# Attention rebuilt for a mixture-of-experts kernel: r and k loaded column-first, scores of a head pair on two 64-row halves of the array, x stationary in the gate

## The reference

```python
for t in range(S):
    cur = einsum('bhd,bhe->bhde', u * k[t], v[t])
    y[t] = einsum('bhd,bhde->bhe', r[t], state + cur)
    state = w * state + einsum('bhd,bhe->bhde', k[t], v[t])
```

## Time and profile before

| | us |
|---|---|
| median of 3 runs | 2269.34 (2267.15 to 2274.19) |
| the profiled execution, its span | 2269.7 |
| attention, to the first transfer of routing | 211.7 |
| TensorE busy in the first 212 us | 189.2 |
| VectorE, GpSimd, ScalarE busy there | 136.4, 105.3, 32.8 |

### The profile page before, as it was taken

How to read it: one execution, slowest core, us unless ns; L and a number is a source line. 1 busy time by engine, 2 the same in 40 slices (tenths; PEclk the granted TensorE clock), 3 DMA queues, 4 the chain that set the end, 5 groups by cost and what they waited for, 6 DMA issues and landing times.

```text
span 2269.7 us, 31806 instructions
## 1 busy us (share of the span) xinstructions
PE 2104.9 (93%) x12371; PEld 1901.0 (84%) x12371; DVE 819.8 (36%) x1525; ACT 470.7 (21%) x662; POOL 406.3 (18%) x258
## 2 busy tenths in 40 slices
PE   6996333999989999999999999999999999999998
PEld 6995322999978998998898899899899899889888
DVE  6676776222253223223223223222322322322322
ACT  0112000344412122113112211211221221212211
POOL 4555112555510011002000100200020020003011
PEclk9998555999999999999999999999999999999999
DMA  6453100233310001001000100100010000000000
GB/s 138 79 83 100 51 0 10 79 131 131 122 56 0 0 12 44 0 0 56 0 0 0 55 0 0 55 0 0 0 55 0 0 31 25 0 0 14 17 24 28
DMA packets 105473, 79.33 MB, mean 35 GB/s; under 512 B 77408, under 2 KB 96992, under 8 KB 105440
## 3 DMA queue, kind: packets, MB, share of 16 engines
q1 hardware_dynamic: 102368, 69.44, 11.1%
q0 software_dynamic: 3072, 9.44, 1.2%
HBM read 69.43 MB, written 9.44 MB: 35 GB/s over the span
## 4 chain that ended last, share of the span: by engine, by line
PE 71%; DVE 1%; issue 0%; POOL 0%; DVEq 0%
PE bank L1000 71%; DVE weight L1332 0%; PE bank L972 0%; PE bank L1215 0%; DVE row_sum L1318 0%; DVE x_lo L993 0%; PE bank L984 0%; DVE weight L1321 0%; DVE col_part L1323 0%; POOL out_dram L1307 0%; DVE row_sum L1320 0%; DVE col_inv L1328 0%; DVE col_inv L1331 0%; DVE x_rows L1362 0%; DVE row_sum L1319 0%
## 5 line engine op out<-in xcount | busy, mean ns | idle before, releaser
L1000 PE MATMUL bank<-x_hi,w_hi 128*128 128x512 f32 (+1 forms) x1344 | 524.2, 390 | 1.9 <-ACT x_hi L1079 1.2
L1000 PE MATMUL bank<-x_hi,w_lo 128*128 128x512 f32 (+1 forms) x1344 | 523.8, 390 | 0.0
L1000 PE MATMUL bank<-x_lo,w_hi 128*128 128x512 f32 (+1 forms) x1344 | 520.4, 387 | 0.0
L1000 PE MATMUL bank<-w_hi,h_hi 128*128 128x384 f32 x1536 | 519.4, 338 | 0.0
L1000 PE MATMUL bank<-w_hi,h_lo 128*128 128x384 f32 x1536 | 518.8, 338 | 0.0
L1000 PE MATMUL bank<-w_lo,h_hi 128*128 128x384 f32 x1536 | 518.8, 338 | 0.0
L1279 ACT ACTIVATE h_hi<-bank 128x512 fp32r<-128x512 f32 x384 | 229.7, 598 | 1190.3 <-PE bank L1000 1190.3
L1338 DVE SCALAR_TENSOR_TENSOR h_lo<-bank,h_hi 128x512 fp32r<-128x512 f32 x384 | 265.6, 692 | 557.6 <-ACT h_hi L1279 557.6
L144 POOL TENSOR_TENSOR w_lo<-w_raw,w_hi 128x3072 fp32r<-128x3072 f32 x16 | 109.3, 6831 | 1310.6 <-ACT w_hi L136 1310.6
L1362 DVE SCALAR_TENSOR_TENSOR x_rows<-bank,weight,x_rows 128x384 f32 (+1 forms) x192 | 118.4, 618 | 530.2 <-PE bank L1000 530.2
L1000 PEld LDWEIGHTS bank<-x_hi,w_lo 128*128 128x128 f32 x1344 | 253.9, 189 | 53.5
(11 more groups left out here) (193 smaller groups left out, 1519.3 us busy)
## 6 DMA issues: line engine op xcount, KB each, us to landing
w_raw<-moe_w_dram SPq DMA_DIRECT2D x32, 1536.0 KB, 6.7
r_in<-r_dram SPq DMA_DIRECT2D x24, 192.0 KB, 3.2
k_in<-k_dram SPq DMA_DIRECT2D x24, 192.0 KB, 3.9
v_in<-v_dram SPq DMA_DIRECT2D x24, 192.0 KB, 4.1
x_dram<-x_rows SPq DMA_DIRECT2D x1, 4608.0 KB, 15.0
x_in<-x_dram,home POOLq DMA_INDIRECT x24
out_dram<-x_rows,home POOLq DMA_INDIRECT x24, 2.6
u_tok<-u_dram SPq DMA_DIRECT2D x1, 192.0 KB, 4.5
```

The source lines that it names most:

```text
L1000: done = nc.tensor.matmul(out_tile, a, b, start=first and n == 0, stop=last and n == len(terms) - 1, skip_group_check=True)
```

## The change

Layout. The inputs are laid out anew before the launch, by copying and padding alone: r and k once column-first per chunk (`rk_turned`: per partition, which is a column of a head pair, 2 x 4 x 128 numbers, 4096 bytes) and r, k, v once by rows (`rkv_rows`: per position 3 x 384 numbers, 4608 bytes), w by columns, u repeated for all 128 rows, and gates and expert weights with all that goes to one partition in one run (12 KB for an expert's w1 or w2). Each chunk's tile is two transfers, four buffers deep.

Work. No transposes of r and k. GpSimd scales r in place by decay (`scale_r`), VectorE scales k in place by growth (`scale_k`), one copy. Scores contract over 64 rows: head 0 of a pair on partitions 0 to 63, head 1 on 64 to 127, into different PSUM banks, alternating by head. y and the outer product have 48 and 96 columns per head and pair. The state is kept decayed: the key table contains the chunk's decay, ScalarE scales the old state (`keep_state`, four operations), VectorE adds the outer product per half (`next_state`). A batch's last chunk makes no outer product. x goes straight to x_rows, from there to the transposes, and each chunk's x is stored to x_dram at once. In the gate x is stationary (128x128) and gate1 moves (8 columns), so that logits come out by position. The hardware loop is unrolled; the weights of the first expert load at chunk 12. `loads(t)` is 16 * (t // 4 + 1), and `outers` and `scalings` count the chunks before t that have an outer product or a scaling. Most of the removed lines are those of the functions above; indentation is cut.

```diff
-    SLOTS = 3
+    SLOTS = 4
...
-sp.dma_start(w1_raw[:], src[e].rearrange("(t p) f -> p t f", p=P)).then_inc(w1_loaded, 16)
+sp.dma_start(w1_raw[:], src[e]).then_inc(w1_loaded, 16)
...
+    rkT = sb(ctx, "rkT", [P, SLOTS, 2, HP, P])
+    rows_in = sb(ctx, "rows_in", [P, SLOTS, 3, DM])
+    score_ps = [banks[0:2], banks[2:4]]
+    y_ps = banks[4][:, 0:DM]
+    outer_ps = banks[5][:, 0:DM]
...
+        def load_tile(t):
+            need(sp, x_ready, t - SLOTS + 1)
+            sp.dma_start(rkT[:, t % SLOTS], rk_turned[t]).then_inc(rkT_loaded[t % SLOTS], 16)
+            sp.dma_start(rows_in[:, t % SLOTS], rkv_rows[t]).then_inc(rows_loaded[t % SLOTS], 16)
+        def store_tile(t):
+            sp.wait_ge(x_ready, t + 1)
+            sp.dma_start(x_dram[t * P:(t + 1) * P, :], x_rows[:, t]).then_inc(x_stored, 16)
+        sp.dma_start(w_col[:], w_cols).then_inc(w_loaded, 16)
+        load_tile(0)
+        sp.dma_start(u_tok[:], u_rows).then_inc(u_loaded, 16)
+        load_tile(1)
+        load_tile(2)
+        load_tile(3)
+        sp.dma_start(gate1[:], moe_w_gate).then_inc(gates_loaded, 16)
+        sp.dma_start(gate2[:], moe2_w_gate).then_inc(gates_loaded, 16)
+        for t in range(SLOTS, T):
+            load_tile(t)
+            store_tile(t - SLOTS)
+            if t == T // 2:
                 load_w1(sp, 0, moe_w1, 0)
                 load_w2(sp, 0, moe_w2, 0)
+        for t in range(T - SLOTS, T):
+            store_tile(t)
...
+        def scale_r(t):
+            pool.wait_ge(rkT_loaded[t % SLOTS], loads(t))
+            nc.gpsimd.tensor_tensor(rkT[:, t % SLOTS, 0], rkT[:, t % SLOTS, 0], decay[:, :, 0:P], ALU.mult)\
+                .then_inc(r_scaled, 1)
+        def keys(t):
+            pool.wait_ge(rows_loaded[t % SLOTS], loads(t))
+            need(pool, outer_ready, outers[t - 1] if t > 1 else 0)
+            nc.gpsimd.tensor_tensor(k_tok[:, t % 2, :, 0:D], head_rows(t, 1), growth_tok[:, :, 0:D], ALU.mult)\
                 .then_inc(k_tok_ready, 1)
+        def own_products(t):
+            pool.wait_ge(rows_loaded[t % SLOTS], loads(t))
+            need(pool, rku_ready, t)
+            nc.gpsimd.tensor_tensor(rk[:], rows_in[:, t % SLOTS, 0], rows_in[:, t % SLOTS, 1], ALU.mult).then_inc(rk_ready, 1)
+            pool.wait_ge(rk_ready, t + 1)
+            need(pool, own_summed, t - 1)
+            nc.gpsimd.tensor_tensor(rku[:, t % 2].rearrange("p h d -> p (h d)"), rk[:], u_tok[:], ALU.mult)\
+                .then_inc(rku_ready, 1)
+        pool.wait_ge(decay_ready, 1)
+        scale_r(0)
+        pool.wait_ge(u_loaded, 16)
         pool.wait_ge(tables_ready, 1)
+        for t in range(T):
+            if t % C < C - 1:
+                keys(t)
+            if t < T - 1:
+                scale_r(t + 1)
+            own_products(t)
...
+        def scale_k(t):
+            dve.wait_ge(rkT_loaded[t % SLOTS], loads(t))
+            nc.vector.tensor_tensor(rkT[:, t % SLOTS, 1], rkT[:, t % SLOTS, 1], growth[:], ALU.mult).then_inc(k_scaled, 1)
+        dve.wait_ge(decay_ready, 1)
+        nc.vector.tensor_tensor(growth_out[:], growth[:], pw[:, 7, :].unsqueeze(2).to_broadcast([P, HP, P]),
+            ALU.mult).then_inc(decay_ready, 1)
+        scale_k(0)
         dve.wait_ge(table_turned, 1)
         nc.vector.tensor_copy(growth_tok[:].rearrange("p h d -> p (h d)"), table_ps[:]).then_inc(tables_ready, 1)
+        def mask(t):
+            need(dve, y_ready, t - 1)
             for hh in range(2):
+                dve.wait_ge(scored, 2 * t + hh + 1)
+                nc.vector.tensor_tensor(scores[:, t % 2, hh],
+                    score_ps[t % 2][hh][:].rearrange("p (q t) -> p q t", q=HP),
+                    later[:].unsqueeze(1).to_broadcast([P, HP, P]), ALU.mult)\
+                    .then_inc(masked, 1)
+        def own_rows(t):
             dve.wait_ge(rku_ready, t + 1)
+            nc.vector.tensor_reduce(own_sum[:], rku[:, t % 2], AX.X, ALU.add).then_inc(own_summed, 1)
             dve.wait_ge(own_summed, t + 1)
+            nc.vector.tensor_tensor(own[:, t % 2], rows_in[:, t % SLOTS, 2].rearrange("p (h d) -> p h d", h=H),
+                own_sum[:].unsqueeze(2).to_broadcast([P, H, D]), ALU.mult).then_inc(own_scaled, 1)
+        def x_tile(t):
             dve.wait_ge(own_scaled, t + 1)
             dve.wait_ge(y_ready, t + 1)
+            nc.vector.tensor_tensor(x_rows[:, t], y_ps, own[:, t % 2].rearrange("p h d -> p (h d)"), ALU.add)\
                 .then_inc(x_ready, 1)
+        def next_state(t):
+            c = t % C
+            dve.wait_ge(outer_ready, outers[t + 1])
+            if c > 0:
+                dve.wait_ge(state_scaled, scalings[t + 1])
+            for hh in range(2):
+                part = slice(hh * HW, (hh + 1) * HW)
+                outer = outer_ps[part, :].rearrange("p (q h d) -> p q h d", q=HP, h=2)[:, :, hh]
                 if c == 0:
+                    last = nc.vector.tensor_copy(state[part, (c + 1) % 2, :, hh], outer)
                 else:
+                    last = nc.vector.tensor_tensor(state[part, (c + 1) % 2, :, hh], outer, state_kept[part, :, hh], ALU.add)
+                last.then_inc(state_ready, 1)
+        for t in range(T):
+            mask(t)
+            if t < T - 1:
+                scale_k(t + 1)
+            if t > 0:
+                x_tile(t - 1)
+            if t % C < C - 1:
+                next_state(t)
+            own_rows(t)
...
+        def scores_of(t):
+            pe.wait_ge(r_scaled, t + 1)
+            pe.wait_ge(k_scaled, t + 1)
+            need(pe, masked, 2 * (t - 1))
+            for q in range(HP):
+                for hh in range(2):
+                    part = slice(hh * HW, (hh + 1) * HW)
+                    last = nc.tensor.matmul(score_ps[t % 2][hh][:, q * P:(q + 1) * P], rkT[part, t % SLOTS, 1, q],
+                        rkT[part, t % SLOTS, 0, q], start=True, stop=True)
+                    if q == HP - 1:
+                        last.then_inc(scored, 1)
+        def outer_of(t):
+            pe.wait_ge(k_tok_ready, outers[t + 1])
+            pe.wait_ge(rows_loaded[t % SLOTS], loads(t))
+            need(pe, state_ready, 2 * outers[t])
+            for q in range(HP):
+                last = nc.tensor.matmul(outer_ps[:, q * 2 * D:(q + 1) * 2 * D],
+                    k_tok[:, t % 2, 2 * q:2 * q + 2, :].rearrange("p h d -> p (h d)"),
+                    rows_in[:, t % SLOTS, 2, q * 2 * D:(q + 1) * 2 * D], start=True, stop=True)
+            last.then_inc(outer_ready, 1)
+        def y_of(t):
+            c = t % C
+            pe.wait_ge(rows_loaded[t % SLOTS], loads(t))
             need(pe, x_ready, t)
+            if c > 0:
+                pe.wait_ge(state_ready, 2 * outers[t])
             pe.wait_ge(masked, 2 * t + 2)
-            if c > 0:
-                pe.wait_ge(state_ready, t)
             for q in range(HP):
                 if c > 0:
-                    nc.tensor.matmul(y_ps[:, q * P:(q + 1) * P], rT[:, c % 3, q],
+                    nc.tensor.matmul(y_ps[:, q * 2 * D:(q + 1) * 2 * D], rkT[:, t % SLOTS, 0, q],
                  state[:, c % 2, q].rearrange("p h d -> p (h d)"),
                  start=True, stop=False, skip_group_check=True)
                 for h in (2 * q, 2 * q + 1):
-                    last = nc.tensor.matmul(y_ps[:, h * HW:(h + 1) * HW], scores[:, c % 2, h % 2, q], v_in[:, c, h],
+                    last = nc.tensor.matmul(y_ps[:, h * D:(h + 1) * D], scores[:, t % 2, h % 2, q],
+                        rows_in[:, t % SLOTS, 2, h * D:(h + 1) * D],
                         start=(c == 0), stop=True, skip_group_check=True)
             last.then_inc(y_ready, 1)
...
+        def gate(t):
             pe.wait_ge(xT_ready, t + 1)
-            pe.wait_ge(gates_loaded, 32)
             for d in range(DT):
-                last = nc.tensor.matmul(logitT_ps, gate1[:, d], xT[:, c % 2, d], start=(d == 0), stop=(d == DT - 1))
+                last = nc.tensor.matmul(logit_ps[:, t * E:(t + 1) * E], xT[:, t % 2, d], gate1[:, d],
+                    start=(d == 0), stop=(d == DT - 1), skip_group_check=True)
             last.then_inc(logit_ready, 1)
...
+        pe.wait_ge(decay_ready, 2)
         for q in range(HP):
+            last = nc.tensor.transpose(table_ps[:, q * P:(q + 1) * P], growth_out[:, q], ident[:])
         last.then_inc(table_turned, 1)
+        pe.wait_ge(gates_loaded, 32)
         pe.wait_ge(tables_ready, 1)
         for t in range(T):
+            scores_of(t)
+            if t % C < C - 1:
+                outer_of(t)
+            if t > 1:
+                turn_x(t - 2)
+            if t > 0:
+                y_of(t - 1)
+            if t > 1:
+                gate(t - 2)
+        turn_x(T - 2)
+        y_of(T - 1)
+        gate(T - 2)
+        turn_x(T - 1)
+        gate(T - 1)
...
+        def keep_state(t):
+            act.wait_ge(state_ready, 2 * outers[t])
+            for q in range(HP):
```

(23 more changed lines are left out.)

306 lines of the change are left out of this document (61 added, 245 removed).

## The result

| | us |
|---|---|
| changed kernel, median of 20 runs | 2250.31 (2225.92 to 2325.01) |
| kernel before, median of 20 runs | 2270.35 (2267.15 to 2274.19) |
| ratio, 95% interval | 0.9886 (0.9869 to 0.9902) |
| profiled execution of the changed kernel, its span | 2250.78, 2248.7 |
| attention in it, to the barrier before routing | 187.9 (before 211.7) |

The change makes the kernel 20 us faster, where 46.5 were forecast, and the time lies outside the range of 2211 to 2243. (The ratio stands for 26 us and not 20, since it leaves the five longest runs out; the median of the other fifteen is 2244.57.) The two kernels also differ in how far their own runs lie apart: 7 us before, 99 after.

The account below looks back on a forecast made before the run. Attention was taken as bound by TensorE's row of instructions: start 26.0, 21 chunks 122.2, queueing 3, tile 13 2, tail 12.0, ending at 165.2 instead of 211.7 us. That gave 2223; range 2217 to 2231, eight in ten 2211 to 2243.

Parts of the forecast that it names:

- Then 21 x 5.82 = 122.2: Attention after the scores of chunk 2: 21 chunks at a mean pitch of 5.82 us, 122.2 us in all.
- the hitch at tile 13: Attention near chunk 13: tile queued behind 3.15 MB of expert weights comes late, between 0 and 5 us, taken as 2.
- stays at 1.2 GHz: TensorE's clock remaining at the lower level; sharing a chance of 0.04 with the case of binding transfers.
- tile transfers are hidden: Attention's tile loads: 3.7 us a chunk at near 356 GB/s, hidden behind the work, taken as 0.
- 1.30 + 0.30: Scores in a full chunk: 16 instructions on 64-row halves in 1.30 us, plus 0.30 for changing the array's shape.
- rival D: Scores in attention: pairs of halves overlap fully, -10 us with about 3 given back, 2216; chance 0.15.
- Rival A: Scores in attention: the two halves don't overlap, +11.8 us less 1 of queueing hidden, 2234; chance 0.28.
- first scores released by the gates: Start of attention: TensorE's first scores wait for the gates' transfer, queued behind four tiles and u, until 17.0 us.
- rival C: Attention's transfers bind at 161 GB/s, 8.1 us a chunk, slower than before at 2289; chance 0.04 shared with a low clock.
- rival B: Attention: the path shared by GpSimd and VectorE binds at 6.6 us a chunk, 2239; chance 0.11.
- The 3 us of queueing: Attention: GpSimd and VectorE getting in each other's way, 0.15 us a chunk over 21 chunks.
- Everything after it equal: Stages from routing on: unchanged in time, the prediction counting as wrong if they move by more than 3 us.

Follow-up runs that it names:

- slots6: Changed kernel with six tile buffers instead of four, nothing else: 2224.45 us, ratio 0.9798.
- outer_all: Changed kernel, but the last chunk of each batch makes its outer product again, results unused: 2243.03 us, ratio 0.9896.
- slots6_gap: slots6 plus three waits of TensorE for the state, before the scores of chunks 7, 13 and 19: 2260.29 us, four runs from 2233.04 to 2278.77.
- best: Changed kernel with six tile buffers, gates loaded right behind tile 0, and 22 unread matmuls before the tables are ready: 2211.0 us, ratio 0.9744.
- thick_gate_gap: slots6_gap with the gate's moving operand 128 columns wide instead of 8, the extra results thrown away: 2223.26 us, ratio 0.979.
- before_gap: Kernel before the change, with a TensorE wait for an earlier x tile added in the second chunk of batches 2 to 4: 2272.53 us, ratio 1.0003.
- best_serial: best_thick with scores ordered by head, all of head 0 and then all of head 1, instead of alternating: 2228.62 us, ratio 0.9808.
- best_thick: best with the gate's moving operand 128 columns wide instead of 8: 2212.55 us, ratio 0.9748.
- serial_thick: slots6 with the 128-column gate and scores ordered by head instead of alternating: 2355.77 us, ratio 1.0381.
- serial: Changed kernel with scores ordered by head, all of head 0 and then all of head 1, instead of alternating: 2354.58 us, ratio 1.0362.

## Why the prediction was wrong, step by step

The forecast put the end of attention at 165.2; it came at 187.9. The difference by stretches, forecast against measured: to the scores of chunk 3, 31.8 and 34.84, +3.0; from there to those of chunk 23, 20 x 5.82 + 5 = 121.4 and 141.3, which is -12.2 for the leaner row and +32.1 for waits and low clock; the tail, 12.0 and 11.7, -0.3. Sum +22.7. With the 2.8 us after attention it is the 25.5 us between a span of 2223.2 and 2248.7. The +3.0 are the low clock too: the scores of chunks 0 to 2 take 1.8 us each, and from those of chunk 0 to those of chunk 3 pass 19.1 us, where 14.8 were forecast; in slots6, with the clock up from chunk 1, it is 14.9.

**The step that failed** is "Then 21 x 5.82 = 122.2", and with it the sentence that the hitch at tile 13 costs 2 us. Both take every instruction at the pace of the rows at 2.4 GHz, and a wait at its own length. The clock stood in the forecast only as one that "stays at 1.2 GHz", within a chance of 0.04. What the runs showed in its place: the clock can fall after short waits of TensorE. With the new row and the 8-column gate, six of the seven places with waits of 0.6 to 2.0 us between chunk 3 and the last scores (in the changed kernel, outer_all and slots6_gap) were followed by a fall, once for 3 us and otherwise for 14 to 34 us. Waits of 0.75 to 1.31 us in chunks 1 and 2 of slots6 and best were followed by none; why is open. The row before had fallen too, once, at 40 to 45 us (in the trace 35.5 to 45.7, behind the wait of 3.4 us); I counted its end as a gain, without asking whether the new row would fall more easily. Slots6 (no waits from chunk 3 to the last scores, 2224), slots6_gap (waits, 2233 to 2279), thick_gate_gap (waits, more columns, 2223) and before_gap (waits in the old row, no effect) show trigger and condition apart. The Trainium skill, "TensorE: Matmul & The Clock Gate", A second HAM failure mode: psum-queue depth-cycling, tells of a bf16 kernel in which TensorE's short and frequent idle times between groups of matmuls make the clock swing. Slots6_gap shows such a swing with as few as three waits of 0.82 us. The row of before, with three waits as long, does not: a rule of idle times alone would have put the clock's loss on both kernels. That a row can be busy for 3.00 us of 3.00 and still stay at 0.50 is what the stretches above show.

**Supply** was the second miss, and the trigger. That tile transfers are hidden held for their rate (up to 410 GB/s in 99 to 102 us of the changed kernel; 356 was taken) but not for their time: GpSimd is the first to need a tile, 18 of 24 come late to it, and after a batch's last chunk, which is short (4.8 us), TensorE has caught up. The sum took the mean of the chunks, in which short ones pay for long ones; a wait looks at the shortest.

**Scores**: forecast 1.30 + 0.30, measured 1.09 with the change of shape. The pairs overlap fully: the 16 loads take 0.97 us from the first start to the last end, eight steps of 0.11 where full rows take sixteen (1.86). That was rival D. Its time, 2216, is near what slots6 gives in its fastest runs (2218.57). The 1.30 came from a row that was misread: the 24 logit transposes of the earlier trace rows straddle a fall of the clock, so that their mean of 0.084 us is one of two paces. In before_gap, where the clock stays up, they take 0.065 each, by which 16 would take 1.0:

```profile
211.89 1.55 PEld L506 LDWEIGHTS bank<-ident,logitT 8*128 8x128 f32 x24 [0.64 <-ACT logitT L523]
```

Rival A (no overlap) is nearly best_serial: 1.52, at 16 us over best_thick, where 11.8 were priced.

**Held**: no transposes of r and k; gate 0.77 (0.67); y 2.68 (2.62); outer 0.86 (0.89); first scores released by the gates, at 15.72 (17.0); the hitch at tile 13, 1.64 + 1.23 us (2) by itself; rival C's transfers did not bind. The two VectorE operations beside GpSimd do stretch, scale_k (L311) from 675 to 1646 ns and own (L333; the instructions of the line: min/median/max ns):

```profile
L333 DVE TENSOR_TENSOR own<-rows_in,own_sum x24: 557/559/1412, 21.1 to 181.6; 128x384 f32<-128x384 f32 x24
```

but the pitch of 5.73 in slots6 shows that this costs nothing: rival B falls. The 3 us of queueing were not there either.

**"Everything after it equal"** missed by 2.8 us, just inside the 3 us named. The search is 3.6 us longer: VectorE and GpSimd meet there in another order, shifted by 0.1 us, and VectorE's operations take 3.4 us more. The prediction had this contention and priced it for attention alone, where it cost nothing.

## What to carry to other kernels

When a change makes TensorE's row leaner, count what the row feeds the array (rows, moving columns), not only its instructions, and then look for each wait of TensorE, above all beside the shortest iteration: here a wait of 0.72 us was followed by 24 us at half the clock. The cures are cheap and can be tried one at a time: earlier transfers (26 us here), columns that cost almost no time (a wide gate, 20 us, of which a part is timing), a TensorE at work before the loop begins (13 us, together with earlier gates). Before a pitch is taken from a row of the trace, look whether the granted clock changes inside it. Runs of one kernel that begin to lie far apart are a sign to look at the clock before anything else.

## What the runs showed of the hardware

- Weight loads on two 64-row halves overlap fully when they alternate: in the changed kernel's chunk 3 the two loads of a pair start 0.007 us apart and the next pair 0.11 later, 16 in 0.97. On one half they follow each other every 0.11 us, as full-height ones do (0.112); by head the 16 take 1.52 and not 1.79 only because the second head's first loads run beside the first head's last three. At the slow pace the step is 0.21 (2.80 for 16).
- Loads of 8 rows by 128 columns are faster: 24 in 1.55 us in before_gap.
- The clock has a memory: the same row stays at the pace of 1.2 GHz for all of attention when TensorE was idle before the first scores (serial_thick, 2355.77) and at 2.4 when it was kept at work there (best_serial, 2228.62).
- Of a VectorE and a GpSimd operation that meet, the one that starts first is hardly held up: in the search 0.34 and 0.76 us when VectorE leads by 0.03, 0.74 and 0.59 when GpSimd leads by 0.06.
- The granted clock in the record is 1.00 until its first change, whatever the pace. All of attention in "serial" is recorded so, up to the step from 330 to 188 ns at 487 us, while the six instructions of a gate take 1.40 us there and 0.75 in slots6. Durations decide:

```profile
15.00:60.00 45.00, 44.15 (x214) 42.68 (x215) 21.04 (x34) 7.43 (x20) 23.65 (x23) 1.00 0.26 88
```
